# Sliding-window attention and two mixtures of experts on one core: probabilities turned by VectorE in squares of 32 from the seventh block on

## The reference

```python
# 1: attention, 4 x 8 heads, 576 positions, head size 64, each position sees itself and the 63 before it
scores = scale * q @ k.T;  scores = where(0 <= rel < 64, scores, -1e9)
attn = exp(scores - max);  attn = attn / (sum(attn) + 1e-09)
x = attn @ v                                  # rearranged to (2304, 512)
# 2: gated layer, 512 -> 1536 -> 512
x = (sigmoid(x @ moe_w_gate) * (x @ moe_w_val)) @ moe_w_out
# 3: top-2 of 8 experts, 512 -> 1024 -> 512
noisy = x @ w_gate + log1p(exp(x @ w_noise)) * noise     # the two best per row, softmax over them
out[rows of e] += weight * (relu(x @ w1[e]) @ w2[e])
```

## Time and profile before

| | |
|---|---|
| median of 3 runs | 1055.52 us |
| profiled execution | 1058.44 us, span 1056.8 us |
| granted TensorE clock, mean | 0.986 |
| PE busy | 1029.5 us (97%), 7455 instructions |
| DVE busy | 392.2 us (37%) |
| ACT busy | 387.8 us (37%) |
| POOL busy | 234.5 us (22%) |
| turn_p, L724, PE | 144 transposes, 270 to 476 ns each |
| copy_pT, L996, ACT, 128 x 512 | 34, 581 ns each |

### The profile page before, as it was taken

The page is one execution under the profiler, slowest core; times in us unless marked ns, Lnnn a source line. Parts: engine busy times, 40 slices in busy tenths (PEclk is TensorE's granted clock), DMA queues, the critical chain, the costliest instruction groups (busy, mean ns, idle before and its releaser), DMA issues. The chain is left out here.

```text
span 1056.8 us, 18749 instructions
## 1 busy us (share of the span) xinstructions
PE 1029.5 (97%) x7455; PEld 940.8 (89%) x7455; DVE 392.2 (37%) x1113; ACT 387.8 (37%) x941; POOL 234.5 (22%) x225
## 2 busy tenths in 40 slices
PE   6999999999999999999999999999999999999994
PEld 5999999999999999999999898799898989898983
DVE  3662343342434334242345434433432424343310
ACT  4553243433424333342344433333333333333310
POOL 2581022021111202111022322211304030312111
PEclk6999999999999999999999999999999999999998
DMA  5662113121211212110224232662616263543312
GB/s 174 205 196 71 31 46 96 52 75 51 81 51 50 62 51 81 51 51 1 100 81 147 69 101 41 184 155 58 163 59 153 88 159 100 140 120 100 60 14 37
DMA packets 48249, 95.28 MB, mean 90 GB/s; under 512 B 9504, under 2 KB 14624, under 8 KB 48160
## 3 DMA queue, kind: packets, MB, share of 16 engines
q1 hardware_dynamic: 35696, 66.22, 19.0%
q0 software_dynamic: 12032, 27.31, 12.7%
q10 hardware_dynamic: 432, 0.52, 0.2%
HBM read 72.35 MB, written 21.68 MB: 89 GB/s over the span
## 5 line engine op out<-in xcount | busy, mean ns | idle before, releaser
L760 PEld LDWEIGHTS bank<-xr,wr 128*128 128x128 f32 x2592 | 326.5, 191 | 9.4 <-issue 0.5
L760 PE MATMUL bank<-xr,wr 128*128 128x256 f32 x2592 | 329.3, 283 | 0.0
L838 PE MATMUL bank<-wr 128*128 128x256 f32 (+1 forms) x1536 | 229.8, 310 | 0.6 <-DVE xr L1373 0.3
L838 PEld LDWEIGHTS bank<-wr 128*128 128x128 f32 x1536 | 226.1, 190 | 1.4 <-DVE wr L1373 0.6
L777 PE MATMUL bank<-wr,hr 128*128 128x512 f32 x648 | 176.5, 407 | 0.0
L1267 DVE SCALAR_TENSOR_TENSOR arena<-arena,bank 128x256 f32<-128x256 f32 x108 | 45.4, 420 | 253.0 <-ACT arena L1015 253.0
L1015 ACT ACTIVATE arena<-bank 128x256 f32<-128x256 f32 x108 | 41.5, 384 | 265.9 <-PE bank L760 265.8
L853 PE MATMUL bank<-wr 128*128 128x512 f32 x576 | 136.3, 393 | 0.0
L777 PEld LDWEIGHTS bank<-wr,hr 128*128 128x128 f32 x648 | 113.7, 188 | 23.2 <-issue 2.2
L853 PEld LDWEIGHTS bank<-wr 128*128 128x128 f32 x576 | 106.6, 188 | 21.5
L601 POOL DMA_INDIRECT out<-arena,tab x34 | 53.4, 1572 | 283.8 <-ACT arena L1094 275.3
(11 more groups left out here) (121 smaller groups left out, 781.5 us busy)
## 6 DMA issues: line engine op xcount, KB each, us to landing
arena<-moe_w SPq DMA_DIRECT2D x64, 512.0 KB, 4.4
arena<-gv SPq DMA_DIRECT2D x12, 512.0 KB, 3.8
out<-zeros POOLq DMA_DIRECT2D x20, 256.0 KB, 2.7
arena<-v SPq DMA_DIRECT2D x18, 256.0 KB, 2.7
x_rows<-arena SPq DMA_DIRECT2D x9, 512.0 KB, 3.1
arena<-v SPq DMA_DIRECT2D x34, 128.0 KB, 2.7
arena<-k SPq DMA_DIRECT2D x17, 256.0 KB, 3.5
arena<-q SPq DMA_DIRECT2D x16, 256.0 KB, 3.6
```

Of the source, the lines that this page charges most:

```text
L760: mm = pe.matmul(o, gv_w[:, f, w, kk], xr[:, g % 2, x, kk], start=(m + kk + n == 0), stop=(kk == KC - 1 and n == 2), skip_group_check=True)
L838: mm = pe.matmul(ps_h[u % 2][:, 0:n], w1_r[e % 2][:, a, kk, f * P:(f + 1) * P], xT[p][:, b, kk], start=(kk + x == 0), stop=(kk == KC - 1 a ...
```

## The change

From block 6 on (`SQUARE = 6`) `turn_p` and `copy_pT` are gone. VectorE moves the probabilities into `pT` itself, with 16 transposes of 32 x 32 squares (each for four heads), half of them in slot 3n - 14 and half in 3n - 13. `values(n)` moves from slot 3n - 13 to 3n - 12, the slot of `scores(n + 2)`, behind them. Waits and the two loads of values follow.

```diff
-    P_LATE = {4: 1, 5: 3, 6: 5, 7: 7}
-    PV_LATE = {4: 2, 5: 4, 6: 6, 7: 8}
-    X_LATE = {4: 3, 5: 5, 6: 7, 7: 10}
-    MIXED_LATE = {3: 3, 7: 4}
+    P_LATE = {4: 1, 5: 3, 6: 5}
+    P_LATE2 = {6: 6}
+    PV_LATE = {4: 2, 5: 4, 6: 7}
+    X_LATE = {4: 3, 5: 5, 6: 8}
+    SQUARE = 6
+    Q4 = P // 4
+    MIXED_LATE = {3: 3, 8: 4}
...
-                elif (t := at_slot(s, 6, -18, TT)) is not None and t > 4:
+                elif (t := at_slot(s, 6, -17, TT)) is not None and t > 4:
                     load_mixed(t)
-                elif (t := at_slot(s, 6, -15, TT)) is not None and t > 3:
+                elif (t := at_slot(s, 6, -14, TT)) is not None and t > 3:
                     load_v(t)
...  scores
-                if n > OPEN:
+                if n > SQUARE + 1:
+                    pe.wait_ge(masked, n)
+                elif n > OPEN:
                     pe.wait_ge(masked, n)
                     pe.wait_ge(pT_done, n - 1)
...  turn_p
-                    pe.wait_ge(masked, min(n + 2, NB))
+                    pe.wait_ge(masked, n + 2)
...  TensorE's slots
-                if (n := stage(s, -14, P_LATE)) is not None:
+                if (n := stage(s, -14, P_LATE)) is not None and n < SQUARE:
                     turn_p(n)
-                if (n := stage(s, -13, PV_LATE)) is not None:
+                if (n := stage(s, -12, PV_LATE)) is not None:
                     values(n)
...  exps
-                if n >= 2:
+                if n >= SQUARE + 2:
+                    act.wait_ge(pT_done, n - 1)
+                elif n >= 2:
                     act.wait_ge(p_turned, n - 1)
                     act.wait_ge(rcp_done, n - 1)
...  ScalarE's slots
-                if (n := stage(s, -14, P_LATE)) is not None:
+                if (n := stage(s, -14, P_LATE)) is not None and n < SQUARE:
                     copy_pT(n)
...  VectorE
+            def turn_squares(n, half):
+                if half == 0:
+                    dve.wait_ge(scaled, n + 1 - OPEN)
+                    dve.wait_ge(pv_done, n)
+                for b in range(2 * half, 2 * half + 2):
+                    rows = slice(b * Q4, (b + 1) * Q4)
+                    for a in range(4):
+                        cols = slice(a * Q4, (a + 1) * Q4)
+                        tr = dve.transpose(pT[cols, :, rows], prob(n)[rows, :, cols])
+                if half:
+                    tr.then_inc(pT_done, 1)
...  VectorE's slots, behind h_low
+                if (n := stage(s, -14, P_LATE)) is not None and n >= SQUARE:
+                    turn_squares(n, 0)
+                if (n := stage(s, -13, P_LATE2)) is not None:
+                    turn_squares(n, 1)
                 if (n := stage(s, -18, S_LATE)) is not None:
                     mask_max(n)
```

## The result

The changed kernel takes 1064.94 us (median of 4 runs, 1064.18 to 1066.22) against 1055.65 before: ratio 1.0089, 95% interval 1.0073 to 1.0104. I had forecast 1045.7 with a range to 1059; the time lies outside it and on the other side.

A forecast was written before the change was run, and what follows sets the result against it. TensorE, issuing without gaps, was taken to bound the stage: 18.7 us given back, less 7.9 of waits at values behind routing and 1.0 in the first group, made 9.8 of gain, 1045.7 us; range 1036.5 to 1059.

The forecast's parts named there:

- TensorE's side: TensorE's slots: 13.5 us from dropped transposes, 5.5 from values sharing a slot with scores, 0.3 taken off: 18.7 given back.
- d: On VectorE, the time from one transpose to the next: 0.28 us taken, 0.21 and 0.29 kept for the range.
- my own formula: Second half ready at 5.04 + 16d behind choose_first, 5.52 + 16d behind slots and weights, against values at 9.10.
- the two pairs: Slot pairs with choose_first or slots and weights after the first half: values wait 0.42 and 0.90, six each, 7.9 us.
- the first group: Slots 5 to 10, where VectorE also splits weights: halves delay values and splits, 1.0 us (0.3 to 1.5).
- halves double beside POOL: Rival for the first group: squares beside POOL's splits take twice as long, 5 us, time 1050; chance 6%.
- Where it is hidden and where not: VectorE's squares against the values: hidden in ordinary pairs with 0.8 us to spare, late behind routing steps, 7.9 us.
- The forecast wait at values after slots and weights: TensorE at values, when slots and weights follow the first half: ready at 10.00 against 9.10, 0.90 us, six times.
- VectorE becomes the bound: Rival: from d = 0.32 on VectorE's lateness eats the gain; 5 us slower at 0.34, 39 at 0.42; chance 17%.
- No wait at all: Rival: transposes overlap, d up to 0.25, routing slots cost under 3 us; at 0.21 gain 18.4, time 1037.1; chance 31%.

The follow-up runs named there:

- the merge alone: The kernel before with the values matmuls and their two loads one slot later, nothing else: 1051.67 us against 1056.53, ratio 0.9958.
- the run with half of the squares: The changed kernel with 4 of the 8 transposes left out in each half: 1038.83 us, ratio 0.9831.
- the run with the ranks read first: The changed kernel with the ranking matmuls in piece 1 and the first two steps of slots ahead of the first half: 1054.82 us, ratio 0.9983.
- 12 squares alone: The changed kernel with a second buffer for the turned operand and 12 of the 16 squares turned: 1045.55 us, ratio 0.9899.
- 12 squares and the routing moved: The changed kernel with 12 of 16 squares turned, a second buffer, ranking in piece 1 and the first two steps of slots moved ahead: 1039.03 us, ratio 0.9839.
- the last run: The changed kernel with squares from block 9 on, blocks 6 to 8 turned by TensorE: 1064.64 us, ratio 1.0071.

## Why the prediction was wrong

**TensorE's side held.** The slots of 4.25 and 5.67 are the forecast ones to 0.01 us, the merge alone measured 4.4 for 5.2, and the run with half of the squares gives back 17.7 of 18.7.

**The size of d** (the distance from one transpose to the next). I took 0.28; it is 0.3125 to 0.316 (2.50 and 2.53 us for eight). With 0.3125 in my own formula the two pairs cost 6 x (32 x 0.3125 - 7.64) = 14.2 us, and the first group, measured, 3.9: the sum would have been 18.7 - 18.1, a time of 1055. So d alone explains why the gain is gone, and not why the kernel is slower. I had gone below the duration that the rows gave (0.29); an instruction on other partitions than the one before keeps its full duration, measured 0.302, and has 0.01 on top. I had priced the first group at 1.0 us. With halves of six squares (1.9 us) slots 7 to 9 cost 15.9 - 14.8 = 1.1 us, with eight (2.5) 3.9: at my d (2.24) it lies between, so the price was too low there as well. Of the 3.9, 1.0 us is a wait of the gate matmuls for a split, which I had named. That halves double beside POOL did not occur; the first one of all in the changed kernel's timeline, beside POOL's split:

```profile
56.87 1.37 POOL L542 TENSOR_TENSOR wr<-arena,wr 128x512 fp32r<-128x512 f32 x1
57.00 2.50 DVE L1268 STREAM_TRANSPOSE arena<-arena 32x128 f32<-32x128 f32 x8
```

**The step that failed is "Where it is hidden and where not".** It named one reader of VectorE's work, the values. But the squares stand in front of routing steps, and TensorE reads those too: the ranking in the very slot of the values (`chosen_done`), and the router's transposes in piece 2 (`rank_read`). Before, VectorE had written what these two read 2.4 us ahead of them. In the group of the earlier trace rows, `chosen` and `run` on VectorE, and the ranking (L812) and the router's transposes (L792) on TensorE:

```profile
335.97 0.18 DVE L1323 TENSOR_TENSOR chosen<-marks 128x16 bf16<-128x16 f32 x1
338.56 0.21 PE L812 MATMUL bank<-chosen,ones 128*128 128x16 bf16 x2
345.80 0.16 DVE L1330 TENSOR_TENSOR run<-run,bank 128x8 f32<-128x8 f32 x1
348.39 0.66 PE L792 MATMUL bank<-ident,arena 128*128 128x128 f32 x4
```

So no row of before shows a wait, but one half of the squares, 2.5 us, is more than this slack. And TensorE now comes to the router's transposes earlier: from the start of piece 1 it was 348.39 - 340.12 = 8.27 us before, and would be 4.26 + 3.03 = 7.29 without the wait, since the turning has left piece 1 and the values piece 2. 2.4 - 2.5 - 1.0 leaves 1.1 us short by this estimate, and the wait measured 0.91. The forecast wait at values after slots and weights (0.90, six times) is measured not there but one slot earlier at the router's transposes, 0.91, six times; the run with the ranks read first put it back where I had it. That the sizes agree is luck: with the measured d my formula gives 5.52 + 16 x 0.3125 - 9.10 = 1.42, but it counted piece 2 at 4.25, and the router's transposes make it 4.71. The ranking's wait came on top: piece 0 is 7.73 with it and 6.85 without, 6 x 0.88 = 5.3 us.

**What no term of mine held is the clock.** In three of six groups TensorE, after waits of 1.1 to 1.3 and 0.76 us with 0.7 us of small matmuls between them, is granted half of its clock for some 3 us. Each costs (8.42 + 5.09) - (7.72 + 4.26) = 1.53 us, 4.6 in all. With the ranking moved, so that the wait of 1.1 us at values stood alone, there was none, and none with 12 squares alone, where the wait at the ranking did.

**The sum as measured**, in slots: -17.5 by TensorE's work, +3.9 first group, +6 x 3.1 = 18.6 in the full groups, +4.6 clock, +0.6 for the last two blocks' values (5.36 for 5.07), together 10.2. Slots 0 to 95 grew by 9.6, and the median by 9.3; the 0.6 between is about one slot of the run with half of the squares, which lasts 6.78 where its like last 6.05. Of the 18.6, 5.3 are the ranking's wait.

**The rivals and the range.** "VectorE becomes the bound" came true in the sign, at a d where it was not to happen; it had the price only for the values. My range was also narrower than its own words: at d = 0.35 the formula takes 6 x (32 x 0.35 - 7.64) = 21.4 us and the first group at least 3, a time of 1061 or more, and 1059 belongs to a d a little under 0.34. The measured 1064.94 lies beyond both. "No wait at all" is what the kernel is with 12 squares and the routing moved.

## What to carry to other kernels

When work is put in front of something on an engine that has slack, list everything behind it in the same two or three slots, and who reads it, not only the reader of the work itself; the first late reader hides the next, and a wait taken away there comes back one slot on. TensorE's savings in a saturated stretch can be read from start to start (17.7 came of 18.7), but the cover they need on another engine must be counted at the worst slot of the period. And before moving work to a slower engine, count what need not be done: a quarter of these squares were zeros.

## What was not expected of the hardware

- A transpose of 32 partitions by 128 fp32 elements on VectorE comes 0.315 us after the one before when it reads or writes other partitions, and 0.19 us after it when it stays: 16 of them are 5.0 us of VectorE for what cost TensorE 0.45 and ScalarE one copy of 0.58.
- Two waits of 1.1 and 0.8 us a short way apart can cost TensorE half of its clock for 3 us (0.50 and 0.59 in the rows above); whether they do varies from group to group and, by the spread of times and granted clocks of the last run, it seems from execution to execution. What decides it stays open.
- The order of small matmuls and full ones matters: leaving and entering the gate matmuls once and not twice in three slots is worth 0.21 us by the rows, and 4.4 us in 26 times, 0.17 each, when measured alone.
